# V rows loaded once and copied across partitions, loops over the batches written out, and a weight preparation moved, in an attention and routed-expert kernel

## The chip, the cores and the metric

The kernel runs on one core of one Trainium2 chip. The metric is the device time of one execution in microseconds. The names of the engines in the rows are PE (TensorE matrix multiplies), PEld (its weight loads), DVE (VectorE), ACT (ScalarE), POOL (GpSimd) and SP (SyncE, which here only issues DMAs; its queue is SPq).

## The reference

Three stages follow each other, all in f32.

```python
# attention: B, H, S, D = 4, 8, 768, 64; chunk 32, left 16, right 8, 8 memory rows
for c in range(S // 32):
    k_full = concat([mem_k, k[:, :, max(0, 32*c - 16):min(S, 32*c + 40)]])   # v the same
    a = softmax(q[:, :, 32*c:32*c + 32] @ k_full.T / 8)
    out[:, :, 32*c:32*c + 32] = a @ v_full
# routed experts: x is (3072, 512), 8 experts of 384 places, D 512, F 1024
logits = x @ w_gate            # pairs (token, expert) are taken in falling order of logit,
                               # each token once, each expert up to 384 tokens
out[mask_e] = relu(x[mask_e] @ w1[e]) @ w2[e]
# dense stage on every row
h = x @ w_in; solu = h * softmax(h); ln = layernorm(solu) * g_ln; out = ln @ w_out
```

## The kernel before, in words

**Attention** works on 24 units of 128 tokens (6 for each of the 4 batches); a unit holds 4 chunks of 32 tokens and all 8 heads, as 4 pairs of heads. One head of a pair lies on partitions 0 to 63, the other on 64 to 127. For K the partitions are the head dimension. For V the 64 partitions of a head are the 64 rows of a chunk's window: 16 left rows, 32 own rows, 8 right rows, 8 memory rows. Windows of neighbouring chunks overlap by 24 rows, and the host writes each chunk's window out in full, so these rows are loaded twice, and the memory rows once for every chunk. A column of ones in V gives the sum of the softmax.

SP loads each unit with two DMAs: Q and K (`load_qk`, L341, 768 KB) and V (`load_v`, L347, 520 KB). The tile `unit` has 3 buffers. `load_qk` waits for the scores of the unit three before it, `load_v` for that unit's `values`; `store` (L353, 256 KB) writes a finished unit to `x_dram`.

TensorE goes through steps (L439). Step i runs `scores(i)` (L393), `probs_T(i-1)` (L403), `gate(i-3)` (L436), `x_T(i-2)` (L429) and `values(i-1)` (L418). ScalarE's step (L688) copies the transposed probabilities (L694), the gate's logits (L698) and the transposed output (L704), and takes the exponential (L708). VectorE runs `soften` (L869: mask, row maximum L882, subtraction L888) and `normalise` (L893: L896, L898, L904). On all four of these engines the first batch's six steps stand one after the other in the program, and the other three batches are a hardware loop (`Fori`) whose body holds six steps.

GpSimd meanwhile prepares w_in and w_out for the dense stage (L1247 to L1272): eight pieces of 512 KB are loaded into the two buffers of `raw`, those of w_out are scaled with g_ln (L1264), and each is split into a high part (L1270) and a low part (L1272).

**Routing** of the first expert follows (`best_open`, `begin_search`, `search`, `choose`): 17 rounds of counting on VectorE with one small matrix multiply each. When the expert is known (`w_idx`, L1009), GpSimd's queue fetches its weights (`fetch_weights`, L1274), which on GpSimd stands behind the preparation. The preparation's end (`prep_lo`) also releases `raw` for these and TensorE's `rows_T` (L669). Then eight experts follow, each with its dense stage, while the next expert is searched.

Of the kernel before, what the change touches and what calls it, by code (L numbers as in the profile page):

```python
# [47 lines left out]
QW, KW, VW = HP * P, HP * CPT * WIN, HP * CPT * (D + 1)  # L48
# [44 lines left out]
def build(nc, unit_in, w_gate, w1, w2, w_in, w_out, g_ln, out):  # L93
    ctx = ExitStack()
    with ctx:
# [97 lines left out]
        logits_ps = sem("logits_ps")  # L193
        dve = sem("dve")
# [56 lines left out]
        unit = sb("unit", [P, 3, QW + KW + VW], F32, attn)  # L251
# [39 lines left out]
        v_of = lambda i: unit[:, i, QW + KW:].rearrange("p (h c d) -> p h c d", h=HP, c=CPT)  # L291
# [14 lines left out]
        O_BANK = [KF % 3, (KF + 1) % 3, (KF + 2 + KD + 2 * TILES) % 3]  # L306

# [24 lines left out]

        block = ctx.enter_context(nc.Block())
# [3 lines left out]
        def _(sp):  # L337
# [3 lines left out]
            def load_qk(u, r, first=False):  # L341
                if not first:
                    sp.wait_ge(scores_ps, u - 2)
                sp.dma_start(unit[:, r % 3, 0:QW + KW], unit_in[bass.ds(u, 1), :, 0:QW + KW]
                             .rearrange("a p n -> (a p) n")).then_inc(qk_loaded[r % 3], 16)

            def load_v(u, r, first=False):  # L347
                if not first:
                    sp.wait_ge(pv_ps, u - 2)
                sp.dma_start(unit[:, r % 3, QW + KW:], unit_in[bass.ds(u, 1), :, QW + KW:]  # L350
                             .rearrange("a p n -> (a p) n")).then_inc(v_loaded[r % 3], 16)

            def store(u, r):  # L353
                sp.wait_ge(x_ready, u + 1)
                sp.dma_start(x_dram[bass.ds(u * P, P), :], x_sb[:, r % 3, :, :, :].rearrange("p a b d -> p (a b d)"))\
                  .then_inc(x_stored[r % 3], 16)

            for u in range(3):
                load_qk(u, u, first=True)
                load_v(u, u, first=True)  # L360
            load_qk(3, 0)
            for u in range(2):
                load_qk(u + 4, u + 1)
                load_v(u + 3, u)
                store(u, u)
            with sp.Fori(0, B - 1) as b:
                for r in range(TPB):
                    load_qk(b * TPB + (r + 6), r)
                    load_v(b * TPB + (r + 5), r + 5)
                    store(b * TPB + (r + 2), r + 2)  # L370
            load_v(NT - 1, TPB - 1)
            for u in range(NT - 4, NT):
                store(u, u)
# [5 lines left out]
        def _(pe):  # L379
            def scores(u, r, n):  # L380
                early = isinstance(u, int) and u < 2
                pe.wait_ge(qk_loaded[r % 3], 16 * n)
                if not early:
                    pe.wait_ge(shifted, u - 1)
                if not (isinstance(u, int) and u < 4):
# [21 lines left out]
            def values(u, r, n):  # L407
                pe.wait_ge(pT_sb, u + 1)
                pe.wait_ge(v_loaded[r % 3], 16 * n)
                if not (isinstance(u, int) and u < 1):  # L410
                    pe.wait_ge(x_ready, u)
                pe.sem_inc(pe_past, 1)
                v = v_of(r % 3)
                for hp in range(HP):
                    for a in range(2):
                        for c in range(CPT):
# [3 lines left out]
                                pT[rows, r % 2, hp, CHUNK * c:CHUNK * (c + 1)], v[rows, hp, c, :],  # L420
                                start=True, stop=True)
# [17 lines left out]
            def step(i, r, n, n_before):  # L439

                known = isinstance(i, int)
                if not known or i < NT:
                    scores(i, r, n)
                if not known or 1 <= i <= NT:
                    probs_T(i - 1, (r - 1) % TPB)
                if not known or i >= 3:
# [957 lines left out]
```

## Time and profile before

| | us |
|---|---|
| median of 3 runs | 838.25 |
| lowest and highest | 837.78, 840.58 |
| profiled execution: own time | 838.25 |
| profiled execution: span from first to last instruction | 836.5 |
| attention: start of the trace to the last gate logits | 0 to 152.6 |
| first routing until the expert is known | 154.3 to 193.9 |
| experts and dense stage | 194 to 836.5 |

The page of the profile gives busy time by engine, the span in 40 slices, the queues and the chain of work that ended last. A view of windows gives, for stretches of time, each engine's busy time with its number of instructions, the granted TensorE clock, the DMA engines' share and the bytes moved. In the timeline, what stands in brackets is the idle time before a row and what ended it; "issue" is idle time that no recorded event ended.

### The profile page before, as it was taken

To read this page: it belongs to the slowest core of one execution; us is meant where nothing else is said; L and a number is where in the kernel's file an instruction comes from. 1 tells how busy PE (TensorE), PEld (TensorE's weight loads), DVE (VectorE), ACT (ScalarE), POOL (GpSimd) and SP (SyncE) were. 2 spreads that over 40 slices of the span, in tenths; PEclk is the share of its full clock that TensorE was granted. 3 is DMA by queue.
4 is the path that set the end of the run, shared out by engine and by line. 5 is a ranking of instruction groups with operands and counts; after the bars stand their busy time and mean duration, and the time that the engine had idled before them with its cause. 6 is when DMAs were issued, how large, how long until landed. Compare 5 with 4: busy or idle time off the path is not lost.

```text
span 836.5 us, 17717 instructions
## 1 busy us (share of the span) xinstructions
PE 713.3 (85%) x6837; PEld 617.2 (74%) x6838; DVE 552.4 (66%) x2135; ACT 315.9 (38%) x521; POOL 334.2 (40%) x243
## 2 busy tenths in 40 slices
PE   4677948411899899999999999999999999999993
PEld 3455736200798789888897988898888979898882
DVE  3344624687677886988798687869877886832140
ACT  2223513102223651463256137415623561473170
POOL 5791000005632761582176147506722751574001
PEclk9778988755799999999999999999999999999997
DMA  8988963004202311330132033213302320331000
GB/s 344 350 298 288 353 246 130 27 0 150 89 1 79 107 55 44 112 122 27 51 116 87 26 89 116 74 52 101 101 26 69 109 76 26 114 114 51 1 13 39
DMA packets 24941, 89.35 MB, mean 107 GB/s; under 512 B 3360, under 2 KB 3360, under 8 KB 24864
## 3 DMA queue, kind: packets, MB, share of 16 engines
q0 software_dynamic: 14208, 50.34, 18.6%
q1 hardware_dynamic: 10656, 37.97, 12.6%
q8 instruction: 50, 0.82, 0.4%
q14 instruction: 27, 0.22, 0.1%
HBM read 75.71 MB, written 12.58 MB: 106 GB/s over the span
## 4 chain that ended last, share of the span: by engine, by line
PE 62%; POOL 9%; issue 9%; DVE 8%; DMA 8%; ACT 2%; SPq 0%; POOLq 0%; DVEq 0%; ACTq 0%
PE bank L503 16%; PE bank L505 15%; PE bank L504 15%; POOL wl L1294 6%; DMA raw<-w,w_idx 5%; PE bank L436 3%; PE bank L393 2%; PE banks L418 2%; DMA unit<-unit_in 2%; PE bank L403 2%; PE bank L429 2%; POOL raw L1288 2%; DVE hits L960 1%; DVE z L1089 1%; DVE hot_a L960 1%
## 5 line engine op out<-in xcount | busy, mean ns | idle before, releaser
L1288 POOL DMA_INDIRECT raw<-w,w_idx x60 | 67.0, 1116 | 284.9 <-DVE w_idx L1009 247.7
L1294 POOL TENSOR_TENSOR wl<-raw,wh 128x1024 fp32r<-128x1024 f32 x60 | 146.8, 2449 | 19.5 <-ACT wh L729 18.3
L503 PE MATMUL bank<-xh,wh 128*128 128x384 f32 x256 | 91.5, 357 | 3.7 <-POOL wl L1294 3.5
L729 ACT ACTIVATE wh<-raw 128x1024 fp32r<-128x1024 f32 x60 | 63.3, 1056 | 82.6 <-DMA raw<-w,w_idx 82.6
L503 PE MATMUL bank<-hh,wh 128*128 128x384 f32 x256 | 90.1, 352 | 0.0
L505 PE MATMUL bank<-xh,wl 128*128 128x384 f32 x256 | 87.3, 341 | 0.0
L504 PE MATMUL bank<-xl,wh 128*128 128x384 f32 x256 | 87.3, 341 | 0.0
L505 PE MATMUL bank<-hh,wl 128*128 128x384 f32 x256 | 86.0, 336 | 0.0
L504 PE MATMUL bank<-hl,wh 128*128 128x384 f32 x256 | 85.9, 336 | 0.0
L503 PE MATMUL bank<-wout_h,uh 128*128 128x512 f32 x192 | 78.5, 409 | 0.2
L503 PE MATMUL bank<-win_h,yh 128*128 128x512 f32 x192 | 77.3, 403 | 0.0
L505 PE MATMUL bank<-wout_h,ul 128*128 128x512 f32 x192 | 75.1, 391 | 0.0
L504 PE MATMUL bank<-wout_l,uh 128*128 128x512 f32 x192 | 75.0, 390 | 0.0
L505 PE MATMUL bank<-win_h,yl 128*128 128x512 f32 x192 | 74.9, 390 | 0.0
L504 PE MATMUL bank<-win_l,yh 128*128 128x512 f32 x192 | 74.8, 390 | 0.0
L960 DVE TENSOR_SCALAR_CACHE_REDUCE hits<-VB,bank 96x256 bf16<-96x256 f32 x137 | 65.7, 479 | 5.0 <-DVE bank L981 0.2
L828 ACT ACTIVATE z<-bank 128x512 f32<-128x512 f32 x48 | 28.7, 598 | 90.5 <-PE bank L505 90.5
L977 DVE SCALAR_TENSOR_TENSOR over<-bank,four 96x3 bf16<-96x3 f32 (+1 forms) x128 | 20.3, 159 | 61.3 <-PE bank L480 59.5
L821 ACT ACTIVATE yh<-bank 128x384 fp32r<-128x384 f32 x32 | 15.7, 492 | 119.3 <-PE bank L505 119.3
L480 PE MATMUL bank<-cnt,same_expert 96*96 96x3 bf16 (+1 forms) x137 | 24.8, 181 | 39.0 <-DVE hot_a L960 35.8
L960 DVE TENSOR_SCALAR_CACHE_REDUCE hot_a<-VB,bank 96x256 bf16<-96x256 f32 x120 | 57.1, 476 | 0.0
L960 DVE TENSOR_SCALAR_CACHE_REDUCE mask<-VB,bank 96x256 bf16<-96x256 f32 x120 | 57.1, 476 | 0.0
(178 smaller groups left out, 1625.9 us busy)
## 6 DMA issues: line engine op xcount, KB each, us to landing
unit<-unit_in SPq DMA_DIRECT2D x24, 768.0 KB, 6.4
unit<-unit_in SPq DMA_DIRECT2D x24, 520.0 KB, 5.4
x_rows<-x_sb SPq DMA_DIRECT2D x24, 256.0 KB, 4.8
raw<-w_in POOLq DMA_DIRECT2D x4, 512.0 KB, 8.3
raw<-w_out POOLq DMA_DIRECT2D x4, 512.0 KB, 6.2
raw<-w,w_idx POOLq DMA_INDIRECT x60, 4.3
gath<-x_rows,ids POOLq DMA_INDIRECT x24, 3.5
out<-z,ids_prev POOLq DMA_INDIRECT x14
```

Of the source, the lines that this page charges most:

```text
L393: mm = nc.tensor.matmul(S_PS[r % 2][a][CHUNK * c:CHUNK * (c + 1), hp * WIN:(hp + 1) * WIN], q[rows, hp, CHUNK * c:CHUNK * (c + 1)], k[rows ...
L436: mm = nc.tensor.matmul(GATE_PS[r % 2], wg[:, k, :], xT[:, r % 2, k, :], start=(k == 0), stop=(k == KD - 1))
L480: nc.tensor.matmul(TOT[0:G, 0:n], same_expert[:, :], cnt[:, 0:n], start=True, stop=True)\
L503: nc.tensor.matmul(bank, stat_h, mov_h, start=first, stop=False)
L504: nc.tensor.matmul(bank, stat_h, mov_l, start=False, stop=False)
L505: return nc.tensor.matmul(bank, stat_l, mov_h, start=False, stop=last)
L729: nc.scalar.activation(wh[:, c % WCH, :], stage(s, c), ACT.Copy).then_inc(w_hi, 1)
L828: nc.scalar.activation(z[:, g // 2, 512 * (g % 2):512 * (g % 2) + 512], MM[z_bank(s, g)][:, :], ACT.Copy)\
L960: ins = nc.vector.tensor_scalar(hits_of[n], VB[:, :], cand[:, n:n + 1].bitcast(F32), None, ALU.is_ge, ALU.add, accum_out=cnt[:, n:n + 1])
L977: done(nc.vector.scalar_tensor_tensor(out=over[:, 0:tries], in0=TOT[0:G, 0:tries], scalar=float(CAP), in1=four[:, 0:tries], op0=ALU.is_ge, ...
L1288: gp.indirect_dma_start(stage(s, c), None, table, bass.IndirectOffsetOnAxis(ap=w_idx[:, c % WCH:c % WCH + 1], axis=0))\
L1294: gp.tensor_tensor(wl[:, c % WCH, :], stage(s, c), wh[:, c % WCH, :].bitcast(F32), ALU.subtract)\
```

## The change

V moves out of `unit` into a ring `vr` of 12 slots, one for a chunk, in the order slot, pair of heads, row. A chunk's 32 first rows on the 64 partitions of a head are now the 32 rows of the token stream that begin 16 before the chunk; the 24 rows that follow are the first 24 rows of the next chunk and are copied from the next slot's partitions. Own rows come with one DMA for each head of the pair (32 partitions each), memory rows with one each (8 partitions), and only in the first three units of a batch, because they stay in the slots. VectorE copies for one head of the pair, ScalarE for the other (`next_front`), one unit ahead of `values`. A 25th load brings one slot of padding. The loops over the batches are written out on all engines. GpSimd begins the preparation of w_in and w_out when the last loads of attention have landed.

```diff
+RING = 3 * CPT
-        unit = sb("unit", [P, 3, QW + KW + VW], F32, attn)
+        unit = sb("unit", [P, 3, QW + KW], F32, attn)
+        vr = sb("vr", [P, RING, HP, D + 1], F32, attn)
...
+        def next_front(engine, copy, a, u):
+            if u == 0:
+                engine.wait_ge(v_loaded[0], v_count(0))
+            engine.wait_ge(v_loaded[(u + 1) % 3], v_count(u + 1))
+            if u >= 3:
+                engine.wait_ge(pv_ps, u - 2)
+            own, after = slice(64 * a, 64 * a + FRONT), slice(64 * a + CHUNK, 64 * a + CHUNK + FRONT)
+            s = CPT * (u % 3)
+            if s + CPT < RING:
+                last = copy(vr[after, s:s + CPT, :, :], vr[own, s + 1:s + CPT + 1, :, :])
+            else:
+                copy(vr[after, s:RING - 1, :, :], vr[own, s + 1:RING, :, :])
+                last = copy(vr[after, RING - 1, :, :], vr[own, 0, :, :])
+            last.then_inc(v_next[a], 1)
...
-            def load_v(u, r, first=False):
-                if not first:
+            def load_v(u):
+                if u >= 3:
                     sp.wait_ge(pv_ps, u - 2)
-                sp.dma_start(unit[:, r % 3, QW + KW:], unit_in[bass.ds(u, 1), :, QW + KW:]
-                             .rearrange("a p n -> (a p) n")).then_inc(v_loaded[r % 3], 16)
+                slots = slice(CPT * (u % 3), CPT * (u % 3) + (CPT if u < NT else 1))
+                for a in range(2):
+                    if u % TPB < 3 and u < NT:
+                        sp.dma_start(vr[64 * a + 64 - MEM:64 * a + 64, slots, :, :].rearrange("p c h d -> p (c h d)"),
+                                     v_mem[u // TPB, a, :, :]).then_inc(v_loaded[u % 3], 16)
+                    own = vr[64 * a:64 * a + CHUNK, slots, :, :].rearrange("p c h d -> p (c h d)")
+                    sp.dma_start(own, v_in[u, a, :, 0:own.shape[1]]).then_inc(v_loaded[u % 3], 16)
...
+            load_qk(0)
+            load_qk(1)
+            load_v(0)
+            load_v(1)
+            load_qk(2)
+            load_v(2)
+            load_qk(3)
+            for u in range(NT):
+                if u + 4 < NT:
+                    load_qk(u + 4)
+                if u + 3 <= NT:
+                    load_v(u + 3)
                 store(u, u)
...
-            def values(u, r, n):
+            def values(u, r):
                 pe.wait_ge(pT_sb, u + 1)
-                pe.wait_ge(v_loaded[r % 3], 16 * n)
+                for a in range(2):
+                    pe.wait_ge(v_next[a], u + 1)
...
-            for i in range(TPB):
-                step(i, i, i // 3 + 1, (i - 1) // 3 + 1)
-            with pe.Fori(1, B) as b:
-                for r in range(TPB):
-                    step(b * TPB + r, r, b * 2 + (r // 3 + 1), b * 2 + ((r - 1) // 3 + 1))
-            for i in range(NT, NT + 3):
-                step(i, i % TPB, 0, NT // 3)
+            for i in range(NT + 3):
+                if i < NT:
+                    scores(i, i % TPB)
...
     # ScalarE, after the exponential of step i
+                    next_front(act, lambda to, of: nc.scalar.activation(to, of, ACT.Copy), 1, i)
...
     # VectorE
+            for u in range(NT):
+                soften(u, u % TPB, 2 * (u // TPB) + (1 if u % TPB == 0 else 2))
+                if u >= 1:
+                    normalise(u - 1, (u - 1) % TPB, None if u - 1 < 3 else (u - 1) // 3)
+                next_front(ve, lambda to, of: nc.vector.tensor_copy(to, of), 0, u)
...
     # GpSimd
             gp.wait_ge(small_in, 32)
+            for i in range(3):
+                gp.wait_ge(qk_loaded[i], 16 * (NT // 3))
+            gp.wait_ge(v_loaded[0], v_count(NT))
             prep_load(0)
```

## Rows read from the trace of the kernel before

**Rows 1.** Chain of waits, 0 to 220 us: shares of that stretch by line.
```profile
by line: issue 19.5%; PE bank L436 12.7%; PE bank L393 9.4%; PE banks L418 8.7%; DMA unit<-unit_in 7.3%; PE bank L403 7.3%; PE bank L429 7.2%; DVE hits L960 3.8%; DVE hot_a L960 2.8%; DVE mask L960 2.8%; POOL z L1288 2.4%; PE bank L480 2.0%
```
**Rows 2.** View of windows, one for each batch of attention.
```profile
core 0: us, PE busy (x) PEld busy (x) DVE busy (x) ACT busy (x) POOL busy (x), PEclk, DMA share, GB/s
6.24:40.90 34.66, 22.47 (x760) 17.11 (x762) 13.78 (x44) 9.45 (x18) 21.14 (x20) 0.88 0.97 374
41.50:78.70 37.20, 27.95 (x864) 20.30 (x864) 15.71 (x52) 11.87 (x24) 22.94 (x15) 0.80 0.87 298
79.37:103.30 23.93, 23.89 (x864) 18.04 (x864) 15.46 (x51) 11.48 (x24) 0.00 (x0) 0.93 0.92 333
110.55:145.40 34.85, 27.23 (x858) 19.73 (x864) 14.92 (x48) 11.85 (x24) 0.00 (x0) 0.84 0.51 171
```
**Rows 3.** Timeline of PE: start, us, line, count, idle before and its releaser.
```profile
24.18 0.97 PE L393 MATMUL bank<-unit 64*32 64x64 f32 x49 [4.41 <-issue]
...
110.60 1.17 PE L393 MATMUL bank<-unit 64*32 64x64 f32 x64 [7.27 <-issue]
...
141.00 0.34 PE L418 MATMUL banks<-unit,pT 64*32 64x65 f32 x13 [0.84 <-issue]
```
**Rows 4.** View of windows, cut where idle time named "issue" ended; the last is the routing.
```profile
0.00:15.49 15.49, 4.94 (x221) 3.97 (x221) 4.33 (x14) 3.08 (x4) 6.76 (x29) 1.00 0.83 325
15.49:63.63 48.14, 33.77 (x1000) 24.60 (x1001) 18.49 (x60) 13.58 (x27) 41.05 (x30) 0.78 0.91 332
63.63:78.44 14.81, 11.87 (x375) 8.76 (x374) 6.82 (x22) 5.93 (x12) 1.94 (x1) 0.89 0.87 291
110.55:132.27 21.72, 15.94 (x457) 11.32 (x458) 8.01 (x26) 5.94 (x12) 0.00 (x0) 0.75 0.57 189
132.27:145.19 12.92, 11.09 (x375) 8.21 (x374) 6.91 (x22) 5.70 (x12) 0.00 (x0) 1.00 0.42 144
154.30:193.90 39.60, 5.32 (x22) 3.35 (x21) 30.84 (x176) 0.00 (x0) 0.00 (x0) 0.52 0.00 0
```
**Rows 5.** DMA queues from 5 to 79 us, then all from 79.37 to 103.3.
```profile
q0 software_dynamic: 1152, 4.19, 14.8%
q8 instruction: 12, 0.20, 1.0%
...
q1 hardware_dynamic: 2174, 7.98, 92.4%
```
**Rows 6.** Who waited on SP's queue; both unit loads on the page; their landing times.
```profile
SPq L350 <- PE banks L418: 60.5, 21, 7.1
...
unit<-unit_in SPq DMA_DIRECT2D x24, 768.0 KB, 6.4
unit<-unit_in SPq DMA_DIRECT2D x24, 520.0 KB, 5.4
...
DMA to landing us min/median/max: 3.3/5.9/12.2
```
**Rows 7.** Groups by line: copies and similar work on DVE, then two on ACT.
```profile
L956 DVE COPY VB<-bank 96x256 f32<-96x256 f32 x1 | 0.4, 412 | 0.8 <-issue 0.8
L950 DVE TENSOR_SCALAR mask<-mask 128x192 f32<-128x192 f32 x1 | 0.3, 260 | 0.0
...
L694 ACT ACTIVATE pT<-bank 128x512 f32<-128x512 f32 x24 | 14.3, 597 | 69.5 <-PE bank L403 69.5
L729 ACT ACTIVATE wh<-raw 128x1024 fp32r<-128x1024 f32 x60 | 63.3, 1056 | 82.6 <-DMA raw<-w,w_idx 82.6
```
**Rows 8.** Timeline of POOL: the preparation, and what follows it.
```profile
15.97 1.03 POOL L1270 CAST win_h<-raw 128x1024 fp32r<-128x1024 f32 x1 [7.75 <-DMA raw<-w_in]
...
20.31 1.05 POOL L1270 CAST win_h<-raw 128x1024 fp32r<-128x1024 f32 x1
...
37.12 3.12 POOL L1264 TENSOR_SCALAR raw<-raw,gain 128x512 f32<-128x512 f32 x2 [1.03 <-DMA raw<-w_out]
...
63.23 2.34 POOL L1272 TENSOR_TENSOR wout_l<-raw,wout_h 128x1024 fp32r<-128x1024 f32 x1
...
194.88 1.07 POOL L1288 DMA_INDIRECT raw<-w,w_idx  x1 [129.31 <-DVE w_idx L1009]
```

More of the change, by code:

```diff
@@ L90, in rounds_in, with build @@
     return ROUNDS_NONE if last else ROUNDS_FIRST if first else ROUNDS
-def build(nc, unit_in, w_gate, w1, w2, w_in, w_out, g_ln, out):
+def build(nc, qk_in, v_in, v_mem, w_gate, w1, w2, w_in, w_out, g_ln, out):
     ctx = ExitStack()
@@ L193, in build @@
         logits_ps = sem("logits_ps")
+        v_next = [sem(f"v_next{a}") for a in range(2)]
         dve = sem("dve")
@@ L339, in _, with load_qk @@
             sp.dma_start(gain[:, :], g_ln).then_inc(small_in, 16)
[L341 to L342 removed]
+            def load_qk(u):
+                if u >= 3:
                     sp.wait_ge(scores_ps, u - 2)
[L344 to L348 removed]
+                sp.dma_start(unit[:, u % 3, :], qk_in[u, :, :]).then_inc(qk_loaded[u % 3], 16)
@@ L353, in store @@
             def store(u, r):
                 sp.wait_ge(x_ready, u + 1)
-                sp.dma_start(x_dram[bass.ds(u * P, P), :], x_sb[:, r % 3, :, :, :].rearrange("p a b d -> p (a b d)"))\
+                sp.dma_start(x_dram[u * P:u * P + P, :], x_sb[:, r % 3, :, :, :].rearrange("p a b d -> p (a b d)"))\
                   .then_inc(x_stored[r % 3], 16)
[L358 to L361, printed above, removed]
@@ L379, in _, with scores @@
         def _(pe):
[L380 to L383, printed above, removed]
+            def scores(u, r):
+                pe.wait_ge(qk_loaded[r % 3], 16 * (u // 3 + 1))
+                if u >= 2:
                     pe.wait_ge(shifted, u - 1)
-                if not (isinstance(u, int) and u < 4):
+                if u >= 4:
                     pe.wait_ge(gate_sb, u - 3)
@@ L419, in values @@
                                 PW[CHUNK * c:CHUNK * (c + 1), a, hp * (D + 1):(hp + 1) * (D + 1)],
-                                pT[rows, r % 2, hp, CHUNK * c:CHUNK * (c + 1)], v[rows, hp, c, :],
-                                start=True, stop=True)
+                                pT[rows, r % 2, hp, CHUNK * c:CHUNK * (c + 1)],
+                                vr[rows, CPT * (u % 3) + c, hp, :], start=True, stop=True)
                 mm.then_inc(pv_ps, 1)
@@ L437, in gate @@
                 mm.then_inc(gate_ps, 1)
[L439 to L446, printed above, removed]
-                    gate(i - 3, (r - 3) % TPB)
-                if not known or 2 <= i <= NT + 1:
-                    x_T(i - 2, (r - 2) % TPB)
-                if not known or 1 <= i <= NT:
-                    values(i - 1, (r - 1) % TPB, n_before)
             pe.wait_ge(consts, 1)
             pe.wait_ge(small_in, 32)
-            for i in range(TPB):
-                step(i, i, i // 3 + 1, (i - 1) // 3 + 1)
-            with pe.Fori(1, B) as b:
-                for r in range(TPB):
-                    step(b * TPB + r, r, b * 2 + (r // 3 + 1), b * 2 + ((r - 1) // 3 + 1))
-            for i in range(NT, NT + 3):
-                step(i, i % TPB, 0, NT // 3)
+            for i in range(NT + 3):
+                if i < NT:
+                    scores(i, i % TPB)
+                if 1 <= i <= NT:
+                    probs_T(i - 1, (i - 1) % TPB)
+                if i >= 3:
+                    gate(i - 3, (i - 3) % TPB)
+                if 2 <= i <= NT + 1:
+                    x_T(i - 2, (i - 2) % TPB)
+                if 1 <= i <= NT:
+                    values(i - 1, (i - 1) % TPB)
             pe.wait_ge(gate_sb, NT)
```

102 lines of the change are left out of this document (44 added, 58 removed).

## The prediction

> **What bounds the kernel now.** The change touches attention and the start of routing, so the chain of waits is read first for that stretch [rows 1]. Its largest entry is not an engine but "issue", 19.5% of 220 us, some 43 us: the chain sits on TensorE while nothing recorded holds it. Loads of units are 7.3%, VectorE's attention work does not appear. Next come the batches one by one [rows 2]. All have nearly the same 864 matrix multiplies and 864 weight loads (a few records missing, and the first batch is cut at the loop), but the third takes 23.93 us and the others 34.66, 37.20 and 34.85. The third has PE busy without a break. It is not the one with idle DMAs: their share is 0.92. So data loads do not set the pace; SP's queue itself waited 60.5 us for `values` to free a V buffer [rows 6], so loads run ahead.
>
> The timeline shows what does: TensorE stops in the middle of a group, after 15 of 64 multiplies of `scores` for 4.41 us, or after 51 of 64 of `values` for 0.84 us [rows 3]. No semaphore stands there. Cut at such stops, the windows hold 749, 915, 2001 and 749 PE instructions [rows 4], which is 3, 3.7, 8 and 3 times 250. The one cut that starts elsewhere is the 915, at the loop's start. The instruction queue moved 12 packets of 16 KB from 5 to 79 us, and none from 79.37 to 103.3, the fast batch; there the unit queue is alone [rows 5]. I read this as: TensorE's code arrives in blocks of about 250 recorded instructions, requested late, and it stops where a block is late. The second turn of the loop finds its code in place. The third turn does not, and its jump costs 7.27 us [rows 3].
>
> The Trainium skill says the same of the form (Runtime: NRT & Kernel Launch, section Instruction fetch mechanics): TensorE's instruction memory of 128 KiB is a FIFO filled in 16 KiB blocks, a taken branch breaks the prefetch, and it prefers full unrolling. The trace agrees on the branch into the fourth batch, and disagrees on the one into the third, which cost nothing and saved every fetch; by the page alone, unrolling only gains.
>
> **A price for a block** [rows 4]. While w_in and w_out load (15.49 to 63.63): 48.14 us / 8 = 6.02 us. Without them, loads going on: 14.81 / 3 = 4.94 us, and 21.72 / 3.66 = 5.93 us in the stretch that restarts after the jump with a slow clock (0.75 granted, between the levels 1.2 and 2.4 GHz). With few loads left (DMA 0.42): 12.92 / 3 = 4.31 us. Without any fetch the third batch does 250 instructions in 23.93 x 250 / 1728 = 3.46 us. So the DMA load decides how late a block is, between 4.31 and 6.02.
>
> **Part 1, the loops written out.** A step has 1728 / 6 = 288 recorded PE instructions, and all 24 steps now fetch: 6912 in all. By 15.49 us before, 442 were done. I take that point as 14.5, since Q and K of unit 1 no longer stand behind 520 KB of V. The other 6470 are 25.9 blocks, of which 3.5 run after the last Q and K loads at 4.31 = 15.1 us. For the other 22.4 I take 4.9 us, next to the 4.94 of the only loaded stretch that has neither the weight loads nor a jump behind it, as after the change; slightly under it for part 2. Sum: 14.5 + 109.8 + 15.1 = 139.4, where the same point of the program was 145.4 before [rows 2]: **-6.0 us**. In it are the jump (-7.3) and the lost free batch, which at 4.9 takes 6.9 x 4.9 = 33.9 in place of 23.9 (+10.0); the rest comes from batches 1, 2 and 4. The shorter code of a step (register work of the loop) is within the rounding.
>
> **Part 2, less V.** A unit moves 768 + 520 + 256 = 1544 KB now. At 7.98 MB in 92.4% of 23.93 us [rows 5], 361 GB/s, that is 4.4 us of the DMA engines. After, V is 260 KB and 65 KB of memory rows for half the units, in all 1317 KB on average: 3.7 us. At my 4.9 a step is 288 / 250 x 4.9 = 5.6 us, so the DMA share falls to 0.67, from 0.87 in the stretch with 4.94. The rest of the 4.19 MB of weights [rows 5] leaves attention too. These loads are hidden already, so their only worth is through the blocks. Below, nothing is gained; above, every block goes at 4.31.
>
> Against it speaks a page of the Trainium skill (SBUF — State Buffer, section Door 1: The DMA port swizzle): 32 or 64 adjacent partitions reach only 8 of the 16 ports, and two such transfers run one after the other. No run here has a load of fewer than 128 partitions. By that rule V's halves take as long as the whole did, and the memory rows come on top; it is the mechanism of the second rival.
>
> **Part 3, the copies.** 24 partitions x 1040 f32, for which no row exists. VectorE: from the copy of 256 in 412 ns out of PSUM at one element a cycle, upper bound about 1.25 us; from 192 in 260 ns inside SBUF [rows 7], lower bound about 0.6. I take 0.7, both of its sides being in SBUF. ScalarE: between 597 ns for 512 and 1056 for 1024 [rows 7], so 1.07 us, or 1.3 in every third unit, where it is two instructions. Busy per step goes from 15.46 / 6 = 2.6 to 3.3 (3.8 at most) on VectorE, from 1.9 to 3.1 on ScalarE, against a step of 5.6: hidden behind TensorE's fetches. If that cover went and steps were the 4.0 us of the third batch, VectorE's order (normalise, copy, next soften) would add up to the copy itself, 0.3 to 1 us a step.
>
> The copy also waits for V of the unit after, so V is needed one unit earlier. V is issued when `values` ends; ScalarE wants it about one step later, VectorE about 1.4 us after that. Landing took 5.9 us at the median, 12.2 at most [rows 6], against a step of 5.6, and four or two DMAs stand in SP's queue in place of one. Behind a late V wait ScalarE's pT copy and VectorE's `soften`, and TensorE for both. Bounds: zero (a step's slack) and about 1 us a step. I take **+1.5 us** for the whole.
>
> **Part 4, the preparation moved.** It starts when slot 0's last V load lands. That is issued when `values` of unit 21 ends, in the old frame 141.34 [rows 3], and lands 3.3 us later at best [rows 6]: 144.6. Then the first piece, issue and landing, about 4 us. The four w_in pieces go at 20.31 - 15.97 = 4.34 each, the four of w_out took 65.57 - 37.12 = 28.45 [rows 8]: 45.8 us. End: 194.4. GpSimd needs the expert at 193.9 [rows 4], and its first weight fetch then stood from 194.88 on [rows 8]. The cover is the routing's 39.6 us with the DMAs at 0.00, and it is just as long as the work: **+0.5 us**. Between no cost and +4 if the first landings take the median. Everything after waits for this queue, so each us late is one us of the total.
>
> **Sum**: 838.25 (the profiled execution's own time, also the median) - 6.0 + 1.5 + 0.5 = 834.2, say **834**. The experts are untouched.
>
> **The rivals.**
> Rival one, *fetches stop being late*: with the weights and half of V gone every block takes 4.31. 14.5 + 25.9 x 4.31 = 126.1, which is -19.3; with the same +2.0, 821. For it: 4.31 at a DMA share of 0.42. Against: attention would press the loads closer, a share of 3.7 / 5.0 = 0.74. Chance 0.17.
>
> Rival two, *the free batch is lost and nothing replaces it* (slower): its place is TensorE's block boundaries in the units that still load. If a half-width V load holds the DMA engines as long as the full one, blocks go at 5.5, the mean over both loaded stretches without weights (36.53 / 6.66). 14.5 + 22.4 x 5.5 + 15.1 = 152.8, +7.4, and with +2.0, 848. It is slower from 5.1 us a block on, where parts 1 and 2 give -1.5 and no longer pay for +2.0. For it: 6.02 while two queues were full, and the 5.93 after the jump. Chance 0.27. The skill's port rule would make this one.
>
> Rival three, *the preparation or the V one unit earlier becomes the wait*: with blocks as forecast, +4 for a preparation that starts late, +4 for late V: -6 + 8 = 840. For it: the tie of 194.4 with 193.9. Chance 0.13. That the change does not do what it says (the loads not smaller, a loop left) I see no sign of in the diff.
>
> **How the numbers follow.** Forecast 0.43, rivals 0.17, 0.27, 0.13. The forecast's own range, blocks at 4.6 to 5.1, is 827 to 839. A measurement tells no change within about 0.3%, 835.7 to 840.8. Of the forecast some 0.33 lies under it and 0.10 inside; rival one is faster; rival three splits half and half; of rival two 0.02 is within. Faster 0.50, same 0.18, slower 0.32. The range, 820 to 849, holds rivals one and two at their centres.
>
> **What would show it.** Right: 27 or so stops of PE named "issue", at every 250 instructions, in all batches, none of 7 us; step 24 begun near 139; copies on VectorE near 0.7 us; GpSimd idle until about 138 and its last L1272 piece ending within 1 us of `w_idx`. Wrong: a third batch as fast as before, fetch stops that vanish with the lighter loads, V loads of half the bytes landing no sooner, `values` waiting for the copies, or weight fetches long after `w_idx`.

## The result, and the profile after

| | before | after |
|---|---|---|
| median of 20 runs, us | 839.42 | 843.73 |
| profiled execution: own time | 838.25 | 842.02 |
| profiled execution: span | 836.5 | 840.3 |
| TensorE begins to transpose the gate's logits | 152.7 | 154.4 |
| VectorE copies the logits (M) | 154.35 | 157.05 |
| VectorE begins the search (copy to VB) | 157.14 | 162.35 |
| expert known (`w_idx`) | 193.69 | 199.11 |
| first multiply of the first expert | 216.4 | 222.0 |

The ratio after to before is 1.0045, with an interval of 1.0025 to 1.0065: **slower by 0.45%**. It leaves out three of the 40 executions, which were in a slower state, and so differs from the quotient of the two medians (1.0051). The forecast was 0.5% faster (834, range 820 to 849). The range held it, the sign was wrong.

The table shows where to look. When the expert is known the profiled kernel after is 5.4 us behind: 1.7 from attention, 1.0 because the copy of the logits starts late, 2.5 between that copy and the search, 0.2 in the search. From the first multiply of the first expert to the end it is then 618.3 us against 620.1, so 1.8 us come back. Nothing in that stage was changed, and in the fourteen profiles of this case it took between 617.6 and 622.7 us, so these 1.8 us mean nothing.

The chain of waits of after, 0 to 220 us, answers to [rows 1]:

```profile
by line: issue 18.5%; PE bank L461 11.5%; PE banks L443 9.6%; PE bank L418 8.8%; PE bank L428 7.4%; PE bank L454 6.6%; DMA vr<-v_in 6.0%; DVE hits L963 3.8%; DVE hot_a L963 2.8%; DVE mask L963 2.8%; DVE flips L925 2.5%; POOL z L1294 2.4%; P
```

"Issue" is 18.5% of 220 us, 40.7 us, where it was 42.9. So TensorE's stops without a releaser have not gone away. A new name stands at 2.5%: `flips`, 5.5 us on VectorE, which was not on the chain before.

The timeline of PE shows the stops (start, us, line, count, idle before and its releaser). It answers to [rows 3]:

```profile
25.54 1.01 PE L418 MATMUL bank<-unit 64*32 64x64 f32 x50 [4.78 <-issue]
...
90.94 0.42 PE L418 MATMUL bank<-unit 64*32 64x64 f32 x3 [4.07 <-issue]
...
104.07 0.90 PE L418 MATMUL bank<-unit 64*32 64x64 f32 x41 [3.03 <-issue]
```

They now stand in the third batch too, in the middle of groups, and the 7.27 us of the jump is gone, both as forecast. There are 18 of them before the logits, 30.5 us together; in the kernel before there are 15, 34.1 us together. The forecast had wanted 27 or so. Windows cut at such stops answer to [rows 4]; the last is the routing, from the copy of the logits on:

```profile
core 0: us, PE busy (x) PEld busy (x) DVE busy (x) ACT busy (x) POOL busy (x), PEclk, DMA share, GB/s
0.00:16.65 16.65, 5.00 (x221) 3.97 (x221) 5.03 (x15) 4.21 (x5) 5.46 (x27) 1.00 0.87 239
16.65:62.52 45.87, 32.77 (x1005) 23.87 (x1005) 24.49 (x71) 23.21 (x38) 0.00 (x0) 0.93 0.73 234
62.52:85.06 22.54, 19.54 (x628) 14.45 (x627) 15.24 (x46) 13.61 (x23) 0.00 (x0) 0.92 0.75 245
85.06:104.07 19.01, 11.52 (x377) 8.29 (x377) 8.54 (x24) 8.71 (x14) 0.00 (x0) 0.80 0.69 230
104.07:118.78 14.71, 13.09 (x377) 9.60 (x377) 8.55 (x27) 8.39 (x15) 0.00 (x0) 0.79 0.56 173
118.78:129.95 11.17, 6.63 (x253) 4.96 (x252) 6.66 (x18) 4.58 (x7) 0.00 (x0) 1.00 1.00 312
129.95:147.33 17.38, 15.65 (x501) 11.49 (x501) 10.63 (x33) 11.10 (x20) 0.32 (x1) 0.80 0.31 101
156.01:199.10 43.09, 5.32 (x22) 3.37 (x21) 34.45 (x177) 0.00 (x0) 38.92 (x27) 0.52 0.22 74
```

PE and PEld instructions together, over 250, give 8, 5, 3, 3, 2 and 4 blocks. The loaded stretch, 16.65 to 129.95, is 113.3 us for 21 blocks: **5.40 us a block**, where 4.9 was forecast and rival two had 5.5. The last four blocks, with few loads left, took 4.35 each against the 4.31 taken. Over the loaded stretch the DMA share is 0.73; the forecast had expected 0.67 and took a price that belonged to 0.87. Stretch by stretch the price does not follow the share: 5.73 us a block at 0.73, 4.51 at 0.75, 6.34 at 0.69, 4.90 at 0.56 and 5.59 at 1.00. So the prediction's "the DMA load decides how late a block is" holds for the mean at best.

In the routing's row GpSimd is busy for 38.92 us, where it was idle [rows 4]. The timeline of VectorE and GpSimd at the start of routing:

```profile
147.01 1.33 POOL L1254 DMA_DIRECT2D raw<-w_in  x2 [140.45 <-DMA vr<-v_in]
...
151.49 5.64 DVE L925 TENSOR_SCALAR flips<-digits 96x4 int32<-96x4 int32 x17
151.56 1.05 POOL L1276 CAST win_h<-raw 128x1024 fp32r<-128x1024 f32 x1 [3.23 <-DMA raw<-w_in]
152.70 2.35 POOL L1278 TENSOR_TENSOR win_l<-raw,win_h 128x1024 fp32r<-128x1024 f32 x1
...
157.05 2.34 POOL L1278 TENSOR_TENSOR win_l<-raw,win_h 128x1024 fp32r<-128x1024 f32 x1
157.05 0.34 DVE L929 COPY M<-bank 128x192 f32<-128x192 f32 x1
...
157.94 1.65 DVE L951 TENSOR_TENSOR mask<-M,best 128x192 f32<-128x192 f32 x1
...
159.93 1.59 DVE L954 TENSOR_TENSOR Vm<-M,mask 128x192 f32<-128x192 f32 x1
160.25 1.05 POOL L1276 CAST win_h<-raw 128x1024 fp32r<-128x1024 f32 x1
```

The same four VectorE instructions in the timeline of before:

```profile
149.80 1.29 DVE L922 TENSOR_SCALAR flips<-digits 96x4 int32<-96x4 int32 x17
154.35 0.36 DVE L926 COPY M<-bank 128x192 f32<-128x192 f32 x1 [3.27 <-PE bank L466]
...
155.26 0.36 DVE L948 TENSOR_TENSOR mask<-M,best 128x192 f32<-128x192 f32 x1
...
155.95 0.36 DVE L951 TENSOR_TENSOR Vm<-M,mask 128x192 f32<-128x192 f32 x1
```

The reader is to compare durations, not starts. 17 `flips` took 1.29 us and now 5.64; the mask took 0.36 and now 1.65; `Vm` 0.36 and now 1.59. L951 ends at 159.59, 0.20 us after GpSimd's L1278, which ends at 159.39. L954 ends at 161.52, 0.22 us after the cast, which ends at 161.30. The copy of M out of PSUM begins while L1278 runs and takes its 0.34. The reduction `best` (L950), which reads only M in SBUF, ran from 157.43 beside the same L1278 and took 0.48, as before. So these two instructions with two inputs in SBUF finish when GpSimd's own instruction does. That is the shape of what the Trainium skill says (SBUF — State Buffer, section Who interferes with whom): VectorE and GpSimd share a pair of SBUF ports, an instruction with two SBUF inputs contends for it with a GpSimd instruction that reads SBUF, and whichever issues second blocks until the other is through. The trace agrees for L951, which began after L1278. For L954 the records don't show the order: it began 0.32 us before the cast and was still the one lengthened. `flips` has one input in SBUF and was lengthened too, which the two-input sentence does not cover. It is a rule the prediction should have weighed and did not.

The preparation's own end was well placed, in the same view:

```profile
195.06 2.34 POOL L1278 TENSOR_TENSOR wout_l<-raw,wout_h 128x1024 fp32r<-128x1024 f32 x1
199.11 0.23 DVE L1012 TENSOR_SCALAR w_idx<-row_base,e_rows 128x4 uint32<-128x4 f32 x1
200.29 1.07 POOL L1294 DMA_INDIRECT raw<-w,w_idx  x1 [2.88 <-DVE w_idx L1012]
```

It ended at 197.4 (forecast 194.4), and GpSimd then stood idle 2.88 us until the expert was known and the fetch could begin. The tie the prediction feared did not bind, because the routing had itself become later.

Last, the copies and V. The view of the tile `vr`, 0 to 160 us (durations in ns, minimum, median, maximum), and who waited for it:

```profile
L724 ACT ACTIVATE vr<-vr x32: 398/958/1070, 12.2 to 148.1; 24x1040 f32<-24x1040 f32 x16, 24x780 f32<-24x780 f32 x8, 24x260 f32<-24x260 f32 x8
L919 DVE COPY vr<-vr x32: 272/682/693, 12.2 to 148.6; 24x1040 f32<-24x1040 f32 x16, 24x780 f32<-24x780 f32 x8, 24x260 f32<-24x260 f32 x8
...
ACT vr L724: 15.2, 9
```

VectorE's full copy took 0.69 (forecast 0.7), ScalarE's 1.07 (1.07). ScalarE stood 15.2 us, nine times, behind a V that had not landed. Some of that reached TensorE. The first `values` in the timeline of PE, after and then before:

```profile
14.05 1.16 PE L443 MATMUL banks<-vr,pT 64*32 64x65 f32 x63 [3.19 <-ACT pT L708]
12.33 1.19 PE L418 MATMUL banks<-unit,pT 64*32 64x65 f32 x64 [0.78 <-ACT pT L694]
```

ScalarE's pT copy stood behind `next_front`, which waited for V of the second unit, so `values` began 1.7 us later. A second such stop, 1.28 us at 123.40, has no counterpart before. In all TensorE waited 4.5 us for pT, where it waited 0.8.

### The profile page after: what moved, and what is told of

Same layout as the page of the kernel before. It is cut to its first block, busy times and chain, and to the rows that moved or that the text cites. A ratio compares the mean times of both kernels' runs of the same rounds, so it can differ in the third digit from the quotient of the medians.

```text
span 840.3 us, 17631 instructions
## 1 busy us (share of the span) xinstructions
PE 714.3 (85%) x6838; PEld 616.9 (73%) x6838; DVE 578.6 (69%) x2167; ACT 344.9 (41%) x553; POOL 332.2 (40%) x243
## 4 chain that ended last, share of the span: by engine, by line
PE 61%; POOL 9%; DVE 9%; issue 9%; DMA 7%; ACT 3%; SPq 1%; POOLq 0%; DVEq 0%; ACTq 0%
PE bank L518 16%; PE bank L520 15%; PE bank L519 15%; POOL wl L1300 6%; DMA raw<-w,w_idx 5%; PE bank L461 3%; PE banks L443 3%; PE bank L418 2%; PE bank L428 2%; PE bank L454 2%; DMA vr<-v_in 2%; POOL raw L1294 2%; DVE hits L963 1%; DVE z L1092 1%; DVE hot_a L963 1%
## 5 line engine op out<-in xcount | busy, mean ns | idle before, releaser
L1254 POOL DMA_DIRECT2D raw<-w_in x4 | 2.4, 612 | 141.0 <-DMA vr<-v_in 140.4
```

## The experiments

Each ratio is against runs of the kernel before on the same chip, with its 95% interval. The kernel after stood at 1.0045 (1.0025 to 1.0065). Medians of different experiments were taken on different chips and are compared through these ratios. A run with one profile tells its stages only roughly. Three kernels with the attention code of after, up to what GpSimd and VectorE do behind it (after, e4, e10), began the transposes of the logits at 154.4, 152.6 and 151.3. So a difference of 3 us in attention in single profiles carries little; the ratios and the durations of instructions carry more.

**e1. Before, with the preparation moved alone.**

```diff
             gp.wait_ge(small_in, 32)
+            for i in range(3):
+                gp.wait_ge(qk_loaded[i], 16 * (NT // 3))
+            for i in range(3):
+                gp.wait_ge(v_loaded[i], 16 * (NT // 3))
             prep_load(0)
```

> The kernel before, with nothing but the preparation of w_in and w_out moved behind the last loads of attention. Theory A (late code blocks set attention, and in the routing GpSimd's preparation holds up VectorE instructions that need the port both share): the eight blocks that took 6.02 us beside the weight loads go at about 5.4, some -5 us; the 17 small instructions at L922 and the two comparisons at L948 and L951 take about 7 us longer, of which about 3.4 show in the time until the expert is known. Total 837 to 839. Theory B (the copies and the earlier need of V ate the gain of the lighter loads, the routing costs nothing): 833 to 835.

Measured: 842.37, ratio 1.0037 (1.0012 to 1.0063). The logits' transposes began at 149.9 in place of 152.7, so attention gained 2.8. From M to VB it took 4.56 where it was 2.79, with `flips` at 3.50 us, the mask at 1.72 and `Vm` at 0.77. `w_idx` came at 192.7, 1.0 earlier. By that the kernel should be 1 us faster, and it is 3 us slower. Its profiled execution took 839.78, less than its median and 1.5 over before's 838.25: 1 us ahead at `w_idx`, then 2.6 us more behind the first expert's first multiply (622.7 us to the end, in place of 620.1), where nothing was changed. What follows is only the direction: moving the preparation gains nothing.

**e2. Before, with the loops written out alone.**

```diff
-            with pe.Fori(1, B) as b:
+            for b in range(1, B):
```

The same on SP, ScalarE and VectorE.

> The kernel before, with nothing but the four loops over the batches written out. Theory A: the stall of 7.3 us at the jump into the fourth batch goes, the third batch takes 33 to 35 us in place of 23.9: +3 us, 842 to 843. Theory B: the loops cost only their jump, so 832 to 835. By the Trainium skill's page Runtime: NRT & Kernel Launch, section Instruction fetch mechanics, written-out code only gains.

Measured: 841.76, ratio 1.0035 (1.0012 to 1.0058). The timeline of its PE where the second turn of the loop and the jump were:

```profile
78.94 0.45 PE L418 MATMUL banks<-unit,pT 64*32 64x65 f32 x27 [2.56 <-issue]
...
93.03 0.30 PE L393 MATMUL bank<-unit 64*32 64x64 f32 x2 [2.96 <-issue]
...
105.84 0.66 PE L393 MATMUL bank<-unit 64*32 64x64 f32 x40 [3.02 <-issue]
```

The third batch now stops like the others and there is no stop of 7 us. The forecast's +10.0 for the lost free batch and -7.3 for the jump make +2.7; the ratio is worth +2.9, and the logits came 3.1 later.

**e3. After, with the preparation back at the start.** The waits of GpSimd on Q, K and V were taken out.

> The changed kernel, with the preparation back at the start of the program. Theory A: the routing gets its 3.4 us back, but the blocks of the first 65 us are later (5.7 to 6.0 us in place of 5.4, +3 to +5), and VectorE's copies, 0.69 us now, take up to 2 us more where they meet GpSimd; total 843 to 847, so no gain over the changed kernel. Theory B: total 839 to 840, the routing's 3.4 us are simply won.

Measured: 845.97, ratio 1.0075 (1.0048 to 1.0103). The logits came at 161.4, 7.0 after those of the kernel after, and from M to `w_idx` it took 39.3 as in the kernel before. So in the changed kernel the preparation during attention seems to cost more than during routing, by about 2.5 us (1.0075 less 1.0045), though the two intervals touch.

**e4. After, with `flips` computed before attention.**

```diff
+            ve.wait_ge(consts, 2)
+            for j in range(SEARCH):
+                nc.vector.tensor_scalar(flips[:, j, :], digits[:, :], ...
             for u in range(NT):
                 soften(u, u % TPB, ...
```

> The changed kernel, with the 17 small instructions that fill flips put ahead of attention on VectorE, where GpSimd is idle. In the changed kernel they took 5.64 us in place of 1.29 and ended 0.7 us after the logits were there. Theory A: 0.7 us less in the routing, 0 to 0.6 us more at the start: 843 to 844. If the lengthened instructions all lie on the critical path, 839.

Measured: 844.16, ratio 1.0049 (1.0018 to 1.0080), no change. M was copied 2.2 us after the transposes began, not 2.7, but the mask then took 2.12 us in place of 1.65. So `flips` alone is worth at most the half microsecond by which M comes sooner; the rest of the sharing moves on to the next instruction.

**e5. Before, with the loops written out and the preparation moved**: the changed kernel without its V part.

> The kernel before with the loops written out and the preparation moved, so the changed kernel without its V part. Against it the changed kernel shows what the copies and the lighter V loads do together. If the three parts simply add (loops +2.4, preparation +3.0 by the two kernels with one of them), 845. Theory A (blocks late by DMA load; V's lighter loads help a little and the copies are hidden): 844 to 846, so V is worth 0 to -2 us where GpSimd is idle, while with the preparation early V cost +4. Theory B (copies and early V are what cost): 840 to 841, under the changed kernel by 3.

Measured: 845.75, ratio 1.0045 (1.0023 to 1.0068), the same as after. The logits came at 154.9, `w_idx` at 199.3; after has 154.4 and 199.1. **In this kernel loading each V row once, with its copies and its earlier wait, is worth nothing either way**, within 0.3%. The profiles suggest that this zero is a sum. TensorE's stops named "issue" before the logits make 36.7 us in e5 and 30.5 in after, which is 6.2 less with the lighter V. Against it after waits 3.7 us longer for ScalarE's pT, and its matrix multiplies are busy for 109.9 us in place of 107.7. Single profiles can't fix these sizes, and no run takes the two effects apart.

**e6. Before, with TensorE's loop cut to two turns** and the last batch written out.

```diff
-            with pe.Fori(1, B) as b:
+            with pe.Fori(1, B - 1) as b:
                 for r in range(TPB):
                     step(b * TPB + r, r, b * 2 + (r // 3 + 1), b * 2 + ((r - 1) // 3 + 1))
+            for r in range(TPB):
+                step((B - 1) * TPB + r, r, (B - 1) * 2 + (r // 3 + 1), (B - 1) * 2 + ((r - 1) // 3 + 1))
```

> The kernel before, with TensorE's loop covering batches two and three alone and batch four written out behind it. Theory A, in the form that the second turn finds its code in place and only the second jump back has to fetch: the third batch stays at 24 us and the 7 us stall before the fourth goes: 832 to 834. Rival C, the code behind the loop is not there either once the second turn is over: a stall of about 7 us at the fall-through, 839 to 840. Rival D, the free turn belonged to the longer loop by chance: third batch 34 us, 843 or more.

Measured: 831.1 (828.55 to 833.31), ratio 0.9886 (0.9864 to 0.9909): **faster than both kernels**, by 1.1 and 1.6%. The timeline of its PE; the rows between these two wait for nothing:

```profile
78.56 0.85 PE L393 MATMUL bank<-unit 64*32 64x64 f32 x64 [0.48 <-issue]
101.13 0.85 PE L393 MATMUL bank<-unit 64*32 64x64 f32 x64 [0.21 <-issue]
```

And the window between them (columns as above):

```profile
78.56:101.13 22.57, 22.35 (x864) 17.34 (x865) 15.61 (x52) 11.72 (x24) 0.00 (x0) 1.00 1.00 382
```

The view of the queues for this window has one queue, that of the units, and no instruction packet:

```profile
q1 hardware_dynamic: 2308, 8.62, 100.3%
```

The free batch is kept: 22.57 us with PE busy for 22.35, while the DMA engines are busy all the time. The fall out of the loop at 101.13 costs 0.21 us where the jump back cost 7.27 [rows 3]. The logits came at 142.6, 10.1 earlier, and the time is 8 to 10 us less. This shows the reading on which the prediction rests: code that has been fetched once need not be fetched again in the second turn, and TensorE's waits for code set the pace of attention.

**e7. After, with the copies cut to one element.** The waits of `next_front` stay; the rows that would be copied hold a constant.

> The changed kernel with each copy cut to one element for each of 24 partitions, the rows behind filled once with ones; waits and loads as they are. It leaves the copied V rows out of the result. Theory A: the copies (0.69 us on VectorE, 1.07 on ScalarE) are hidden beside late blocks: 843 to 844, no change against the changed kernel, at most -1.5. Theory B: 24 x 0.15 to 0.3 us come back, 837 to 840.

Measured: 845.16, ratio 1.0044 (1.0019 to 1.0069), no change. The copies themselves are hidden. Their waits were left in, so this says nothing of a V that lands late.

**e8. After, with V loads of the fourth unit and later cut to a sixteenth in width.**

```diff
+                    wide = CPT * HP * (D + 1) if u < 3 else D + 1
...
-                    sp.dma_start(own, v_in[u, a, :, 0:own.shape[1]]).then_inc(v_loaded[u % 3], 16)
+                    sp.dma_start(own[:, 0:wide], v_in[u, a, :, 0:wide]).then_inc(v_loaded[u % 3], 16)
```

> The changed kernel with the V loads of unit 3 and later cut to one sixteenth of their columns, the DMAs and waits the same in number; the later units use stale V rows, so V is left out of the result from there. The DMA share in attention falls from 0.70 to about 0.55. Theory A: blocks come sooner, mean 4.9 us in place of 5.4 on 18 blocks, -6 to -9: 835 to 838. If the number of DMAs and the Q and K loads make the blocks late, and not V's bytes: 842 to 844.

Measured: 838.42, ratio 0.9985 (0.9959 to 1.0011), some 5 us under after; the logits came at 150.8. So the transfers of V that the change leaves still cost about 5 us: DMA engine time does reach the total. By which path is not shown. TensorE's timeline still has 17 stops named "issue", 31.4 us together against 30.5 in after, so lighter loads alone do not end them. What fell in the profile is the busy time of the multiplies up to the logits, 106.3 us in place of 109.9. (This profile is of an execution of 840.23, over the median.)

**e9. After, with TensorE's loop over batches two and three.** The loop of e6, in the changed kernel, with the other engines written out.

> The changed kernel with TensorE's batches two and three as a loop of two turns again, as in the version of the kernel before that took 831.1 us. Theory A: the free turn comes back, six steps in about 24 to 26 us in place of some 34 (the copies may now show, since TensorE no longer waits for blocks there: VectorE's order allows about 4.0 us a step): -7 to -10 against the changed kernel, 833 to 836. If the copies or V one unit earlier become the bound there (Theory B in its weak form), the free turn takes 30 us and the total is 839 or more.

Measured: 834.09 (829.17 to 840.02), ratio 0.9940 (0.9915 to 0.9965). It gains on after what e6 gains on before, less something: it is 0.5% behind e6 and e12. The timeline of its PE from 78 to 107 us has one stop of a new kind:

```profile
78.02 1.17 PE L419 MATMUL bank<-unit 64*32 64x64 f32 x64 [0.25 <-issue]
96.94 1.06 PE L444 MATMUL banks<-vr,pT 64*32 64x65 f32 x64 [2.47 <-ACT pT L719]
106.64 0.85 PE L419 MATMUL bank<-unit 64*32 64x64 f32 x64 [0.22 <-DVE pr L906]
```

The window from the first of these rows to the last:

```profile
78.02:106.64 28.62, 25.93 (x864) 19.44 (x865) 20.40 (x61) 18.14 (x32) 0.00 (x0) 0.84 0.81 261
```

And the timeline of ScalarE and VectorE just ahead of it:

```profile
95.02 1.16 ACT L735 ACTIVATE vr<-vr 24x780 f32<-24x780 f32 x2 [3.04 <-DMA vr<-v_in]
95.02 0.76 DVE L930 COPY vr<-vr 24x780 f32<-24x780 f32 x2 [2.31 <-DMA vr<-v_in]
```

V landed late, the copies waited for it on both engines, ScalarE's pT copy stood behind, and TensorE's `values` behind that. The free batch took 28.6 us in place of 22.6. Of the 6.0 us, this stop is 2.5, and 3.6 are busy time: 25.93 us for the same 864 multiplies that e6 did in 22.35. The granted clock was 0.84 here, between the two levels, and 1.00 in e6, which fits the longer busy time; why it was lower no run shows. So V wanted one unit earlier shows where TensorE does not wait for code; in after it showed at the start.

**e10. After, with the preparation held back until `best_open` is done.**

```diff
             gp.wait_ge(v_loaded[0], v_count(NT))
+            gp.wait_ge(vm_ready, 1)
             prep_load(0)
```

> The changed kernel, the preparation started only when the routing's first comparisons (best_open) are done. Theory A: these instructions return to 0.36 us each and flips to 1.3, the time from the copy of the logits to the expert known goes from 42.1 back to 39 to 40 us; but the preparation then ends 7 to 9 us after the expert is known, so the first weight fetch waits for it: total 848 to 851. If something else than the shared work lengthened them, they stay at 1.6 us and 5.6 us.

Measured: 852.06, ratio 1.0155 (1.0117 to 1.0193). Its timeline of VectorE and GpSimd, against the rows of after above:

```profile
148.45 1.29 DVE L925 TENSOR_SCALAR flips<-digits 96x4 int32<-96x4 int32 x17
153.01 0.36 DVE L929 COPY M<-bank 128x192 f32<-128x192 f32 x1 [3.27 <-PE bank L481]
...
153.91 0.36 DVE L951 TENSOR_TENSOR mask<-M,best 128x192 f32<-128x192 f32 x1
...
154.60 0.36 DVE L954 TENSOR_TENSOR Vm<-M,mask 128x192 f32<-128x192 f32 x1
...
193.72 0.66 DVE L1012 TENSOR_SCALAR w_idx<-row_base,e_rows 128x4 uint32<-128x4 f32 x1
...
203.67 5.33 POOL L1279 TENSOR_TENSOR wout_l<-raw,wout_h 128x1024 fp32r<-128x1024 f32 x1
209.17 1.20 POOL L1295 DMA_INDIRECT raw<-w,w_idx  x1 [0.17 <-POOL wout_l L1279]
```

GpSimd begins only at 155.66. With it idle, `flips`, the mask and `Vm` are back at 1.29, 0.36 and 0.36: that GpSimd's instructions lengthen them is shown. M to VB is 2.78 again. The price stands at the other end: the preparation ends at 209.0, 15 us behind `w_idx`, and the weight fetch with it. Even then, M to `w_idx` was 40.7, 1.4 over before.

**e11. Before, with each V load as two DMAs of 64 partitions**, the same bytes.

```diff
-                sp.dma_start(unit[:, r % 3, QW + KW:], unit_in[bass.ds(u, 1), :, QW + KW:]
-                             .rearrange("a p n -> (a p) n")).then_inc(v_loaded[r % 3], 16)
+                for a in range(2):
+                    sp.dma_start(unit[64 * a:64 * a + 64, r % 3, QW + KW:], unit_in[bass.ds(u, 1), 64 * a:64 * a + 64, QW + KW:]
+                                 .rearrange("a p n -> (a p) n")).then_inc(v_loaded[r % 3], 16)
```

> The kernel before with each V load as two DMAs, for partitions 0 to 63 and 64 to 127; bytes as before. It tests the price of half-width loads: in the changed kernel a packet of 4160 bytes took 218 ns at the median where the kernel before shows 161. If a transfer of half the partitions goes at about half the rate (the Trainium skill's page SBUF — State Buffer, section Door 1: The DMA port swizzle), the packets take 215 to 300 ns, V holds the DMA engines up to 60% longer, and the total rises by 3 to 8 us, 843 to 848. If width doesn't matter, packets stay near 161 ns and the total at 839 to 841.

Measured: 853.6, ratio 1.0214 (1.0162 to 1.0266). That is +14 in the medians, and 18 by the ratio, where +3 to +8 was expected. The queues of four kernels, 62 to 132 us (packets, MB, share of 16 engines), before:

```profile
q1 hardware_dynamic: 5280, 19.43, 78.6%
```

after:

```profile
q1 hardware_dynamic: 4773, 16.07, 70.7%
```

e11:

```profile
q1 hardware_dynamic: 5082, 18.05, 88.5%
```

and e8:

```profile
q1 hardware_dynamic: 4800, 12.81, 55.3%
```

Per MB this is 2.83 us of the 16 engines before (70 us x 0.786 / 19.43), 3.08 after and 3.43 in e11. The change saved 17% of the bytes of this stretch and 10% of the engine time. The records of single packets in the trace, which none of the views lists, say which: a packet of 4160 bytes of V took 161 ns at the median before (128 partitions), 218 in after (32 partitions) and 262 in e11 (64 partitions). From 5 to 150 us V's packets held the engines for 37.7 us before and 26.6 after, a mean over 16: 29% less, for 44% fewer bytes. The packets of Q and K, the same 3072, held them for 49.8 us before and 56.2 after, so the saving in all is smaller still. The Trainium skill's rule (SBUF — State Buffer, section Door 1: The DMA port swizzle) has loads of 32 or 64 partitions reach half the ports. The durations agree in direction; the packets are 1.35 and 1.63 times as long, not twice.

In e11 even the free batch stopped once, for a load of Q and K and not for code, and the jump behind it cost more:

```profile
110.07 0.85 PE L394 MATMUL bank<-unit 64*32 64x64 f32 x64 [1.78 <-DMA unit<-unit_in]
122.66 1.17 PE L394 MATMUL bank<-unit 64*32 64x64 f32 x64 [8.80 <-issue]
```

The logits came 13.5 us later than before. TensorE waited 15.9 us in five places for loads of Q and K, where it was 8.3 in three, and 36.8 us under the name "issue" in place of 34.1. So most of what waiting adds here is data that comes late, not code.

**e12. e6, with the preparation moved as in e1.**

> The kernel before with the two-turn loop and the preparation moved. It asks what moving the preparation is worth where the rest is best. Theory A: attention -3 to -5, routing +2 to +3, total 829 to 832, no gain over the 831.1 of the two-turn loop alone. If the moved preparation costs 3 us for itself, as the kernel with nothing but it (842.4) suggests, 834.

Measured: 829.9 (828.3 to 832.08), ratio 0.9886 (0.9858 to 0.9915), the same as e6 within 0.4%. Against e6's profile the logits came 2.7 earlier (139.9 for 142.6), M 0.9 later behind them, and M to VB took 5.61 for 2.77: `w_idx` 184.7 for 183.6. Moving the preparation gives attention 2.7 us and takes 3.8 from routing.

## Why the prediction was wrong

**What bounds attention** was read rightly. That TensorE waits for its code, that the second turn of the loop needs no fetch, that the third does and pays 7 us: e2 and above all e6 bear it out. Of the signs that the forecast named, stops in all batches and none of 7 us came true. That unrolling only gains did not hold: written-out loops alone cost 0.35% (e2).

**Part 1, the loops, was right in its two terms and wrong in the sum.** +10.0 and -7.3 were measured together as +2.9 (e2). But "the rest comes from batches 1, 2 and 4", some -8.7 us to make -6.0, rested on blocks at 4.9. Measured, the weights' leaving gave attention 2.8 us (e1), 2.7 (e12 against e6), 0.9 (e5 against e2) and 7.0 (after against e3), each from single profiles, and less V nothing (e5 against after). **The step that failed is the price of a loaded block**, 4.9 us in the sum, where 5.40 was measured. It was taken from one stretch of 14.81 us that came out at 4.94 [rows 4], "slightly under it for part 2". The profile after shows 5.40 over 21 blocks, and 5.73 (45.87 / 8) in the very stretch that the weights had left, where 6.02 stood with them. The mean over all loaded stretches without weights, 5.5, was in the prediction as rival two's price, and it was the better estimator: 36.5 us of trace against 14.8.

The point that the sum put at 139.4 came at 147.33 in the profile, 7.9 later. At its 22.4 blocks the wrong price alone would have made 11. Two smaller errors lie beside it. The start took 16.65 us where the sum had 14.5, because the first `values` waited for V of the second unit. And 6912 counts all 24 steps as full, while the first ones do only part of the work: the windows hold 6722 up to that point, 25 blocks instead of 25.9, which is luck worth some 4 us.

**Part 2, less V, was rival two's condition, half met.** "If a half-width V load holds the DMA engines as long as the full one": it held them 29% less. The forecast wanted the DMA share at 0.67 with a block of 4.9; it was 0.73, at 5.40. By e8 the rest of V was still worth 5 us, and by e5 what the change took away was worth nothing that can be measured, net of part 3. Part of what less V could give went to packets that are longer at 32 partitions. That this is all of it was not shown: no run loads the smaller V through all 128 partitions.

**Part 3, the copies and V earlier, +1.5,** can't be judged as a sum. e7 shows the copies hidden, and their durations were as forecast. The second half of the step, V one unit earlier, is real: 15.2 us of ScalarE waiting, nine times, of which TensorE felt two stops, 3.7 us more than e5 has. Most of the rest lay under TensorE's own stops. How much of the 3.7 us reached the total is not shown, as no run takes the earlier wait out. In e9, with the free batch kept, it came out as a stop of 2.5 us. That was the condition the step named: "if that cover went".

**Part 4, the preparation, +0.5,** asked only when it would end. Its cost was elsewhere: "the cover is the routing's 39.6 us with the DMAs at 0.00" looked at the DMAs and at GpSimd's queue, and not at what GpSimd's instructions do to VectorE's beside them. Measured in the profile: M late by 1.0 and M to VB +2.5, with 0.2 in the search 3.7 in place of 0.5; the first two undone in e10. This is the second step that failed: a cost that the sum left at nothing without a reason. None of the rivals had this mechanism. What attention gained by the move is counted under part 1; e12's time against e6's says that gain and loss cancel there. Of rival three, the preparation that ends late did not happen: 2.88 us of idle GpSimd stood behind it. Its late V did, in part.

**The sum, redone with measured terms:** loops +2.9 (e2), V with its copies and waits 0 (e5 against after). The moved preparation came out differently in each surrounding: +3.1 us alone (e1), +0.8 beside written-out loops (1.0045 for e5 against 1.0035 for e2), 0 beside the two-turn loop (e12 against e6), and -2.5 with the new V (after against e3). The second of these is the change's own surrounding but for V, and gives +3.7 us together, against the 3.8 that the ratio gives. Each term carries about 0.2% or 2 us to either side, so the agreement is no proof; what the ratios show clear of noise is that written-out loops cost and nothing else paid for them.

**Left open.** e1 is slower than before by 0.37%, though its profile has it 1.0 ahead at `w_idx`; e12, the same edit on another loop, shows no loss. Why the third turn fetches again and the second does not was not taken apart. Nor was the granted clock in e9's free batch, the spread of a block's price between 4.51 and 6.34 us, or what the lighter V and its earlier wait are worth one without the other.

## What to carry to other kernels

Where the chain says "issue" in a stage of short instructions, count the instructions between the stops before touching data: here two turns of a loop whose body stays in place, and the last batch written out, gave 1.1%, and full unrolling took 0.35%. When loads are made smaller, look at how many partitions each covers: bytes fell by 17% and engine time by 10%. When work moves to an idle engine, ask which instructions run beside it in the new place and whether that stretch is a chain where every one counts; "it ends in time" is half the question.

## What the runs showed of the hardware that was not expected

- Splitting a load of 128 partitions into two of 64, with the same bytes, made its packets 262 ns in place of 161 and the kernel 2.1% slower (e11).
- V's packets at 32 partitions took 218 ns, less than those at 64 (after, against e11; what else was in flight differed).
- Leaving the loop forward after its second turn cost 0.21 us, the jump back into its third 7.27 (e6, [rows 3]).
- 17 integer operations on 96x4 elements went from 1.29 to 5.64 us when GpSimd split weights beside them, and back to 1.29 without it (e10). A reduction with one input in SBUF beside the same work kept its 0.48. GpSimd's L1279 took 5.33 us in place of 2.34 once, at a time when VectorE was at work behind `w_idx` (e10); which of its instructions held it was not looked into.
